# Attention with scores laid keys-on-partitions, row maxima as a 65th contraction row, and one fp32 product with [v | 1]

## The reference

```python
q_rot, k_rot = rotate(q), rotate(k)            # x1*cos - x2*sin, x1*sin + x2*cos
scores = (1/8) * q_rot @ k_rot.T
scores = scores - max(scores, axis=-1)
attn = exp(scores); attn = attn / (sum(attn, axis=-1) + 1e-09)
x = (attn @ v)                                 # to (2304, 512), heads side by side
h = x @ w_in;  x = (h - tanh(h)) @ w_out       # w_in 512x2048, w_out 2048x512
h = x @ w_in2; out = (h * sigmoid(h)) @ w_out2
```

## Time and profile before

| | |
|---|---|
| median of 3 runs | 1187.12 us (1184.62 to 1188.59) |
| profiled execution: span on the core | 1186.9 us, 18468 instructions |
| from the start to the first score matmul | 23.9 us |
| attention on PE | 23.9 to 359.2 us |
| feed-forward on PE | 359.2 us to the end |
| PE / DVE / ACT / POOL busy | 94% / 51% / 44% / 22% of the span |
| DMA | 50.9 MB, 14.2% of 16 engines |

### The profile page before, as it was taken

The page is one execution under the profiler, slowest core; times in us unless marked ns, Lnnn a source line. Parts: engine busy times, 40 slices in busy tenths (PEclk is TensorE's granted clock), DMA queues, the critical chain, the costliest instruction groups (busy, mean ns, idle before and its releaser), DMA issues.

```text
span 1186.9 us, 18468 instructions
## 1 busy us (share of the span) xinstructions
PE 1118.7 (94%) x6560; PEld 1043.8 (88%) x6560; DVE 610.9 (51%) x969; ACT 521.9 (44%) x1128; POOL 263.0 (22%) x171
## 2 busy tenths in 40 slices
PE   2899999999988899999999999999999999999998
PEld 2778888888868899999999999989998989989897
DVE  5899999999976632322323234762323223232322
ACT  3888989898961232232323232222323222232322
POOL 4556564647145500000000003550000000000000
PEclk9999999999998899999999999989999999999999
DMA  5242423233222300000000000320000000000000
GB/s 174 64 112 68 110 67 106 76 93 89 65 86 84 111 32 1 1 0 0 0 0 0 0 0 29 113 71 1 27 0 27 0 0 27 0 27 0 27 0 27
DMA packets 44493, 50.86 MB, mean 43 GB/s; under 512 B 25376, under 2 KB 25648, under 8 KB 44464
## 3 DMA queue, kind: packets, MB, share of 16 engines
q1 hardware_dynamic: 44464, 50.49, 14.2%
HBM read 36.83 MB, written 4.79 MB: 35 GB/s over the span
## 4 chain that ended last, share of the span: by engine, by line
PE 81%; DVE 6%; DMA 4%; ACT 4%; issue 3%; SPq 1%; POOL 1%; ACTq 0%; DVEq 0%; POOLq 0%
PE ps L557 33%; PE ps L576 17%; PE ps L571 16%; PE ps L443 5%; DMA Vk<-Uk 4%; PE ps L417 3%; PE ps L467 3%; PE ps L468 2%; ACT P L694 2%; PE ps L399 1%; DVE g_l L1029 1%; PE ps L421 1%; DVE negmax L886 1%; DVE pt_l L876 1%; DVE pt_r L881 1%
## 5 line engine op out<-in xcount | busy, mean ns | idle before, releaser
L557 PE MATMUL ps<-xs_h,win_l 128*128 128x384 f32 x768 | 260.7, 339 | 2.7 <-DVE xs_l L946 2.7
L557 PE MATMUL ps<-xs_h,win_h 128*128 128x384 f32 x768 | 259.5, 338 | 0.0
L557 PE MATMUL ps<-xs_l,win_h 128*128 128x384 f32 x768 | 259.2, 337 | 0.0
L822 ACT ACTIVATE g_h<-act 128x384 fp32r<-128x384 f32 x192 | 100.9, 525 | 317.5 <-PE ps L576 133.1
L816 ACT ACTIVATE act<-ps 128x384 f32<-128x384 f32 x192 | 94.4, 492 | 246.0 <-PE ps L557 245.9
L557 PEld LDWEIGHTS ps<-xs_h,win_l 128*128 128x128 f32 x768 | 146.0, 190 | 9.3 <-issue 5.8
L1029 DVE TENSOR_TENSOR g_l<-act,g_h 128x384 fp32r<-128x384 f32 x96 | 85.7, 893 | 130.9 <-ACT g_h L822 130.9
L557 PEld LDWEIGHTS ps<-xs_l,win_h 128*128 128x128 f32 x768 | 145.8, 190 | 3.4
L557 PEld LDWEIGHTS ps<-xs_h,win_h 128*128 128x128 f32 x768 | 145.7, 190 | 0.0
L571 PE MATMUL ps<-g_h,wout_l 128*128 128x384 f32 x384 | 129.9, 338 | 9.1 <-DVE g_l L1029 9.1
L1032 DVE SCALAR_TENSOR_TENSOR g_l<-act,g_h 128x384 fp32r<-128x384 f32 x96 | 60.1, 626 | 139.6 <-ACT g_h L822 139.6
(11 more groups left out here) (79 smaller groups left out, 1926.1 us busy)
## 6 DMA issues: line engine op xcount, KB each, us to landing
Vk<-Uk SPq DMA_DIRECT2D x30, 288.0 KB, 3.7
w_stage<-w_in SPq DMA_DIRECT2D x8, 1024.0 KB, 5.0
w_stage<-w_out SPq DMA_DIRECT2D x8, 1024.0 KB, 5.0
raw_q<-q SPq DMA_DIRECT2D x16, 288.0 KB, 3.8
raw_k<-k SPq DMA_DIRECT2D x16, 288.0 KB, 4.3
out<-ostage SPq DMA_DIRECT2D x5, 768.0 KB, 3.5
vr<-v SPq DMA_DIRECT2D x32, 80.0 KB, 2.8
R<-inverse_sums SPq DMA_DIRECT2D x16, 144.0 KB, 2.7
```

The source lines that it names most:

```text
L557: last = mm(o, w[g][:, kk, c:c + 128], x[:, kk, :], start=(n == 0), stop=(n == 11))
L822: nc.scalar.activation(g_h[f % 2][:, :], act[f % 2][:, :], ACT.Copy, scale=(1.0, 0.5)[L]).then_inc(s_gh, 1)
```

## The change

The layouts of q, k, v are made ahead of the launch (`by_pair`, `v_by_unit`): q and k come transposed, head width on partitions, each also with its halves exchanged for the rotation. The kernel then:

- rotates on POOL in 3 tensor operations of 1152 elements per pair (`rope_scale` two, `rope_add` one) and writes the low parts in one more (`qk_low`); ACT writes the high parts in one (`qk_high`);
- has SP stack the parts by DMA: `stack_high` into `tb` (high parts on partitions 0 to 63, partition 64 for a 65th contraction row), `stack_cross` into `ta` (high over low);
- makes scores twice. `row_scores`: queries on partitions, high parts alone, 20 matmuls of 288 columns per pair, only for `row_max` on DVE. The negated maxima are transposed (`max_transpose`), copied (`copy_rows`) and stored by SP into partition 64 of `tb` (`max_rows`), where the keys' side holds ones. `scores`: keys on partitions, 40 matmuls of 288 columns, which come out with the maximum already taken off. `row_scores` is for the pair ahead, one unit of it before each unit of `scores`;
- `exps` on ACT has no bias and no accumulator and writes P in fp32 where the weighing reads it; there is no transpose of P and there are no parts of it;
- `weigh`: 20 fp32 matmuls of 288 columns per pair, with [v | 1] as stationary operand, so the sums come out beside the weighted values;
- DVE moves the result out (`move_out`), SP gathers the sums, joins the two heads, stores and spreads the inverse; `invert` is on DVE, `normalise` on POOL;
- `stage` now lies over the attention's buffers, so weights 0 and 1 are loaded in pairs 14 and 15 (`load_w`), and weights 2 and 3 after the last `spread_inverse`.

The feed-forward's loops are as before but for names. The diff, cut to its core:

```diff
@@ SP, in order, for each pair n
+            def stack_high(n):
+                if n >= 3:
+                    sp.wait_ge(s_st, 9 * (n - 2))
+                sp.wait_ge(s_hq, n + 1)
...
+                for h in range(2):
+                    sp.dma_start(t[64:65, h, Q, data(h)]..., zrow...to_broadcast([1, 9, 64])).then_inc(s_tb, 16)
+                    sp.dma_start(t[0:64, h, :, data(h)].bitcast(F32),
+                                 hl[64 * h:64 * h + 64, QH:KH + 1:2, :].bitcast(F32)).then_inc(s_tb, 16)
+            for n in range(PAIRS):
+                if n + 1 < PAIRS:
+                    stack_cross(n + 1)          # 4 DMAs of 288 KB, waits s_st, s_lq
+                if n + 3 < PAIRS:
+                    load(n + 3)                 # 1 DMA of 1152 KB
+                max_rows(n, 1)                  # 2 small DMAs, waits s_rw
+                if n >= 1:
+                    gather_sums(n - 1, 1)       # 1 DMA
+                    join_heads(n - 1)           # 1 DMA of 144 KB
+                if n + 2 < PAIRS:
+                    stack_high(n + 2)           # 4 DMAs
+                if n >= 1:
+                    store_inverse(n - 1)        # 1 DMA, waits s_ri
+                    spread_inverse(n - 1)       # 2 DMAs of 144 KB, waits s_scr
+                if n >= 1 and n + 1 < PAIRS:
+                    load_v(n + 1)               # 2 DMAs of 160 KB in pieces of 256 B
+                gather_sums(n, 0)               # 1 DMA, waits s_ev[0]
+                if n + 1 < PAIRS:
+                    max_rows(n + 1, 0)          # 2 small DMAs
+                if n >= PAIRS - 2:
+                    load_w(n - (PAIRS - 2))
@@ PE
-                T, U, V = Tq[pr.par], Uk[pr.par], Vk[pr.par]
+            def row_scores(n, j):
...
+                        last = mm(ps[:, XB + half, 0:HALF], t[0:65, a, Q, unit_cols(a, i)], t[0:65, a, K, c:c + HALF], ...)
+            def scores(n, u, extra=None):
...
+                        last = mm(ps[:, bank + half, 0:HALF], w, x, start=(m == 0), stop=(m == len(terms) - 1))
+            def weigh(n, u, part=None):
...
+                    last = mm(ps[:, OB + half, 0:HALF], v1[n % 2][:, slot, :], P[g % RING][:, HALF * half:HALF * half + HALF],
+                              start=first, stop=final)
+            for n in range(PAIRS):
+                for u in range(9):
+                    if n + 1 < PAIRS:
+                        row_scores(n + 1, u)
+                    extra = None
+                    if u == 0:
+                        extra = (n, 1)
+                    elif u == 6 and n + 1 < PAIRS:
+                        extra = (n + 1, 0)
+                    scores(n, u, extra)
+                    weigh_slot(9 * n + u - 2)
@@ ACT
-                                     bias=negmax[pr.par][:, m:m + 1],
-                                     accum_out=rsum[pr.par][:, m:m + 1]).then_inc(s_exp, 1)
+                nc.scalar.activation(P[g % RING]..., ps[:, bank:bank + 2, 0:HALF],
+                                     ACT.Exp).then_inc(s_ex, 1)
+                    if u == 3 and n + 2 < PAIRS:
+                        qk_high(n + 2)
@@ DVE
+                for u in range(9):
+                    if n + 1 < PAIRS:
+                        row_max(n + 1, u)
+                    if u == 1:
+                        move_out(n - 1, 1)
+                    if u == 4:
+                        invert(n - 1)
+                    if u == 6:
+                        move_out(n, 0)
+                    if n >= PAIRS - 2 and u == 8:
+                        weight_high(n - (PAIRS - 2))
+            n = PAIRS - 1
+            move_out(n, 1)
+            x_low(0, 0)
+            invert(n)
@@ POOL
+            for n in range(PAIRS):
+                if n + 2 < PAIRS:
+                    qk_low(n + 2)
+                else:
+                    weight_low(n - (PAIRS - 2))
+                if n + 3 < PAIRS:
+                    rope_scale(n + 3)
+                if n >= 1:
+                    normalise(n - 1)
+                if n + 3 < PAIRS:
+                    rope_add(n + 3)
```

More of the change, by code:

```diff
@@ L58, in attention_and_two_ffn @@
         shared = cursor[0]
+        stage = [place(f"w_stage{i}", [128, 4, 512]) for i in range(2)]
         xs_h = place("xs_h", [128, 4, TN], F32R)
@@ L71, in attention_and_two_ffn @@
         cursor[0] = shared
[L72 to L90, removed]
@@ L91, in attention_and_two_ffn @@
-        idf = place("idf", [128, 128])
[L92 to L98, removed]
+        raw = [place(f"raw{i}", [128, 4, S]) for i in range(2)]
+        ctab = place("ctab", [128, 2, S])
+        stab = place("stab", [128, 2, S])
@@ new lines, in attention_and_two_ffn @@
+        s_rope = sem("pair_rotated")
+        s_hq = sem("qk_high")
+        s_l0 = sem("first_pair_low")
+        s_lq = sem("qk_low")
+        s_tb = sem("high_tiles_stacked")
+        s_ta = sem("cross_tiles_stacked")
+        s_x = sem("row_scores_done")
+        s_mx = sem("max_done")
+        s_rw = sem("max_rows_copied")
+        s_m = [sem(f"max_rows_stored{h}") for h in range(2)]
+        s_tm = sem("first_max_transposed")
+        s_st = sem("scores_done")
+        s_ex = sem("exp_done")
@@ L155, in attention_and_two_ffn @@
         s_g = sem("gate_split")
-        s_o = sem("down_done")
-        s_ev = sem("down_moved")
+        s_dn = sem("down_done")
+        s_dv = sem("down_moved")
         s_out = sem("out_stored")
[L160 to L173, removed]
@@ L246, in load_w, with spread_inverse @@
+            def spread_inverse(n):
+                sp.wait_ge(s_scr, 16 * (n + 1))
+                if due(n):
+                    sp.wait_ge(s_xm, n)
+                for h in range(2):
+                    one = scratch[n % 2, S * h:S * h + S].rearrange("(a c) -> a c", a=1)
+                    sp.dma_start(R[64 * h:64 * h + 64, :], one.to_broadcast([64, S])).then_inc(s_R, 16)
             def load_w(w):
-                if due(w - 1):
+                if w < 2:
+                    sp.wait_ge(s_lq, PAIRS - 2 + w)
+                else:
@@ L296, in _ @@
-            run_pairs(sp, body)
-            load_w(2)
-            load_w(3)
-            spread_inverse(lambda per: per * PAIRS)
-            for w in range(4, 4 * NG):
+            load_v(1)
+            stack_high(0)
+            stack_cross(0)
+            load(2)
+            max_rows(0, 0)
+            stack_high(1)
+            for n in range(PAIRS):
[19 more added lines that the diff above has]
+                    load_w(n - (PAIRS - 2))
@@ L301, in _ @@
+            n = PAIRS - 1
+            gather_sums(n, 1)
+            join_heads(n)
+            store_inverse(n)
+            spread_inverse(n)
+            for w in range(2, 4 * NG):
                 load_w(w)
             for t in range(NT - 1):
-                sp.wait_ge(s_ev, 4 * NT + 3 * (t + 1))
+                sp.wait_ge(s_dv, 4 * NT + 3 * (t + 1))
                 sp.dma_start(out[t * TN:(t + 1) * TN, :].rearrange("(c p) d -> p c d", p=128),
```

917 lines of the change are left out of this document (329 added, 588 removed).

## The result

The changed kernel takes 1270.41 us (median of 4 runs, 1269.49 to 1271.47) against 1186.3 for the kernel before on the same chip: ratio 1.0706, interval 1.0687 to 1.0724, 7% slower. The prediction was 1184 with a range of 1166 to 1212: wrong in sign and outside the range. The profiled span is 1269.7 us, some 85 us above the prediction, and nearly all of them lie in one place.

What follows compares the result with a forecast made beforehand. PE (19.1 us a pair) and SP's deliveries of maxima (19.3) were taken to bound the attention; 35 + 15 x 19.3 + 28 + 827.7 + 3.7 = 1183.9 us, range 1166 to 1212.

Steps and rivals of the forecast that it cites:

- path (b): `max_rows(n, 1)` on SP behind `stack_cross` and the load: needed 8.5 us into the pair, 0 to 0.4 us late.
- PE's sum: PE's work per pair after the change: 18.6 us, with 0.53 us for each of 20 fp32 `weigh` matmuls.
- R3: Rival: an fp32 matmul costs what the transposes say, 0.25 us; PE 13.0 us a pair, time 1155; chance 0.06, faster.
- R4: Rival: each fp32 matmul shows one uncovered weight load, 0.72 us; PE 22.4 + 0.5, time 1238; chance 0.07, slower.
- The lock: DVE's `invert` waits behind POOL's `qk_low` for shared ports: 0.5 us per pair, or nothing if `invert` comes first.
- Path (a): SP's queue up to `max_rows(n+1, 0)`, needed 0.3 us into the next pair: period at least 19.0 to 20.0 us.
- Start, last pair, feed-forward: First score at 35 us, feed-forward starting 28 us after pair 15 does, then 827.7 + 3.7 us.
- R2: Rival: SP's queue of issues is the bound; period 20.8 us, time 1206; chance 0.25, slower.
- R1: Rival: PE alone sets the period, fp32 matmul 0.49 to 0.51; period 18.0 to 19.0, 1164 to 1179; chance 0.20, faster.
- F: The forecast itself: period 19.0 to 19.7 us, time 1179 to 1190 us; chance 0.42.

Runs made afterwards that it cites:

- the last kernel: `invert` at u = 3 instead of 4, against the kernel where ACT issues the rows behind the exponential: 1171.18 us, ratio 0.9864.

## Why the prediction was wrong

**The step that failed is path (b).** "`max_rows(n, 1)`, needed at 8.5: it stands behind `stack_cross` and the load, 2.3 MB ... about 330 KB per us when full, so it lands at 8.0 to 8.9: 0 to 0.4 us late." The place was right and so was the 8.5, and the size of the landing was wrong: the rows were usable 13.0 us into the pair shown, 4.5 us late, and PE stood 4.9 us on the mean of twelve pairs. The rate came from two landings. From the first issue of `stack_cross`, at 189.98, it took 13.1 us until the load behind it was in, where 2.3 MB at 330 KB per us take 7. The six windows from 191 to 203 give 230 KB per us on the mean, 2.76 MB in all, so some 0.4 MB that SP issues behind the load (by their sizes `join_heads` and the first piece of `stack_high`) went through in the same time.

**Two consequences were not in the sum.** `gather_sums(n-1, 1)` stands in the same queue, so `invert` came 4 us late (hidden while PE waits for rows; visible, at 3.8 us a pair, in the kernel where only the rows were moved). And after each wait PE ran at the lower clock level. In the pair shown the stretch from PE's restart to the next-but-one `weigh` took 4.53 us; in the last kernel the same instructions take 2.84 (195.53 to 198.37), so 1.7 us are lost. That is the least of the twelve: from restart to the end of the pair they take 12.05 to 13.55 us at a mean granted clock of 0.86 to 0.76, and the last kernel 10.38 (195.53 to 205.91) at 1.00. The mean loss is 2.4 us.

**The sum of a pair, now from rows:** 18.74 (PE dense, last experiment) + 4.9 (rows) + 2.4 (clock) = 26.0 us, against 26.2 read for the twelve pairs that wait. `invert` adds nothing to these, as its own wait lies beside PE's. Pair 0 (20.5 us) and the last pairs do not wait and bring the mean of fifteen to 24.9. The cause is thus shown from several sides: by the pairs without a load in the same trace, by removing the load's bytes (−72 us), by moving the load (−50), by moving the rows to another queue and so ahead of the load, which stopped their wait but not that of the sums (−17), and by both together (−80).

**PE's sum came out right in part by luck.** 18.6 us were predicted and 18.74 measured. But 0.53 was taken for an fp32 matmul and 0.49 measured; with 0.49 and 0.134 the sum is 18.0, and the other 0.7 us are two gaps of 0.35 us a pair ahead of a `weigh` that the sum did not have (9.0 us in 26 times; what they wait for is not shown). By the Trainium skill ("FP8 and Floating Point Precision", TensorE Precision Notes) true fp32 goes through the array in four passes; 0.49 is 3.7 times 0.134, so the trace is close to it, a little under. Rival R3, 0.25 each, is out, and so is R4. Only the units are not even: the plain ones take 1.78 us, those with a second group of scores or of `weigh` 2.3 and 3.1.

**The lock was right.** 0.5 us a pair for `invert` behind `qk_low` were forecast, and 0.62 measured once the rows and sums were in time.

**Path (a)** was given as 19.0 to 20.0, and in the changed kernel path (b) hides it. Without the load's bytes the period is 20.3, with 0.6 us of wait at that place: a little over. With the rows issued by ACT it is out of play, and PE sets 19.36.

**Start, last pair, feed-forward.** 35 predicted, 37.87 measured: `row_scores` begins at 21.09, not 20.0, and nine steps of 1.7 us follow, the last at 35.16, where I had five on the path and then the delivery of the maxima; PE then waits 1.87 us for `stack_high(1)`. 28 predicted for the last pair, 27.4 measured, with `x_low` beside `weight_low` as forecast (5.60 us against the 2.1 of the earlier trace rows). 831.4 predicted for the rest, 831.0 measured, and 3.1 us of it went with the weights moved ahead, where the forecast had 3.7 for weight 2. Together 2 us off.

**Rivals.** R2 had the sign, 0.25, and its argument ("at 9 us into the pair the transfers of its first part should have drained") names what failed; but it put the price on SP's issues on path (a), at 1206, and not on what lies in the queue ahead of a small transfer. Its own sum is off too: 19.3 + 1.5 is the lower end, the middle of 1.5 to 2.5 is a period of 21.3 and 1214 us. R1 had the fp32 cost, 0.49, and its 18.0 to 19.0 is the period of the last kernel, but not of this one; R1, F and the range fell with path (b).

**What the idea itself is worth.** With the SP order, one queue, the start, the last pair and the inversion mended, the same arithmetic takes 1171.18 us, 1.4% less than before (interval 1.1 to 1.6%). PE is then the bound at 18.74 us in most pairs, 19.04 on the mean of the first fourteen (35.84 to 302.46), against 20.14 before: some 16 us in 15 pairs. The start takes 13 of them back (first scores at 36.97 instead of 23.9), and as the feed-forward begins at 342.49 instead of 359.2, 16.7 us earlier, the end of the attention gives some 13. Left open: why the burst's rate varies from 171 to 286 KB per us, and how much of the period without the load (20.3) is issue and how much landing; neither was tried separately.

## What to carry to other kernels

Before adding a small transfer whose arrival an engine waits for, write down what stands ahead of it in its own queue, in bytes, and divide by the rate of a burst of just that kind; a mean DMA share of 33 or 56% says nothing about it. Put it in a queue that carries nothing large, or ahead of the large ones, and then look at the next small one in the same queue, which inherits the wait. And read a gap in at least three pairs, and by its total in the waits, before calling it a pattern.

## What the runs showed of the hardware that I had not expected

- A small transfer issued behind large ones in one queue was usable only after them: 2.2 KB, the second part issued at 196.44, 0.44 us after the 1152 KB issued ahead of them, and the sums of the kernel with the rows on ACT's queue, issued at 190.46, 0.18 us after. Issued from ACT's queue ahead of the load, with `stack_cross` under way, the rows were not waited for.
- An fp32 matmul of 288 columns leaves two records, 0.24 us apart, and costs 0.49 us. The distance from its first record to the next instruction's understates it (0.76 us for two), and the two fp32r matmuls behind it show the rest: 0.48 us instead of 0.26.
- The lock between DVE and POOL took an operation of nine elements a partition from 0.16 to 2.54 us; the reciprocal behind it took 0.22 beside either.
- An issue by ACT took 0.53 or 0.62 us as a rule and 1.75 once. Of SP's issues from 189.98 on, the fourth to the seventh, behind three or more large transfers, took 1.29 to 1.47 us, the others 0.6 to 0.8.
